# A three-part kernel in float32: table entries read earlier, the last expert's weights rounded in quarters, the last result in a bank of its own

## What is computed

```python
# experts: B=2, S=768, D=512, E=8, F=1024
for b in range(B):
    prev_e = -1
    for s in range(S):
        fresh_e = int(np.argmax(logits[b, s]))
        e = fresh_e if s == 0 or local_gate[b, s] < 0.5 else prev_e
        prev_e = e
        h = np.maximum(x[b, s] @ w1[e], 0.0)
        out[b, s] = p[e] * (h @ w2[e])
# mixing
theta = x @ w_theta
zr, zi = x * np.cos(theta), x * np.sin(theta)
y = einsum('ts,bsd->btd', w_tok_r, zr) + einsum('ts,bsd->btd', w_tok_i, zi)
u = x + y
out = u + np.maximum(u @ w_ch, 0.0)
```

## Time and profile before

| | us |
|---|---|
| median of 3 runs | 440.62 (440.28 to 440.92) |
| the profiled execution | 440.61 |
| its span, first to last instruction | 438.8 |
| TensorE busy (matmul) | 409.9 (93% of the span) |
| VectorE busy | 254.0 (58%) |
| ScalarE busy | 194.4 (44%) |
| GpSimd busy | 79.1 (18%) |
| mean granted TensorE clock | 0.977 of full speed |

### The profile page before, as it was taken

The page is one execution under the profiler, slowest core; times in us unless marked ns, Lnnn a source line. Parts: engine busy times, 40 slices in busy tenths (PEclk is TensorE's granted clock), DMA queues, the critical chain, the costliest instruction groups (busy, mean ns, idle before and its releaser), DMA issues.

```text
span 438.8 us, 8200 instructions
## 1 busy us (share of the span) xinstructions
PE 409.9 (93%) x2791; PEld 331.4 (76%) x2792; DVE 254.0 (58%) x403; ACT 194.4 (44%) x428; POOL 79.1 (18%) x128
## 2 busy tenths in 40 slices
PE   7779997299999999999999969999999999999997
PEld 3567786157888888888888758888888888888885
DVE  3898885786372624552215656566679465635252
ACT  1777994604264636473317564433333432123010
POOL 3776784121011111111030002500000000000000
PEclk9999999579999999999999989999999999999999
DMA  8999712927434521608140006400000000000012
GB/s 295 403 406 413 271 52 96 410 68 270 189 114 173 164 104 42 239 29 330 49 120 24 2 24 190 129 17 1 1 0 1 24 13 12 24 25 25 24 49 96
DMA packets 12541, 53.96 MB, mean 123 GB/s; under 512 B 1504, under 2 KB 1632, under 8 KB 10848
## 3 DMA queue, kind: packets, MB, share of 16 engines
q1 hardware_dynamic: 7680, 40.46, 23.9%
q0 software_dynamic: 2960, 9.70, 7.0%
q10 hardware_dynamic: 1872, 3.41, 2.0%
HBM read 40.46 MB, written 13.11 MB: 122 GB/s over the span
## 4 chain that ended last, share of the span: by engine, by line
PE 75%; DVE 4%; ACT 2%; issue 2%; ACTq 1%; POOL 1%; DVEq 0%; POOLq 0%
PE ps L1310 15%; PE ps L1312 14%; PE ps L1311 14%; PE ps L1457 7%; PE ps L1459 7%; PE ps L1458 7%; PE ps L1394 2%; PE ps L1358 2%; PE ps L1317 1%; PE ps L1305 1%; PE ps L1208 1%; ACT w_h L674 1%; DVE r_ol L952 1%; DVE w_l L985 1%; ACTq L664 1%
## 5 line engine op out<-in xcount | busy, mean ns | idle before, releaser
L1457 PE MATMUL ps<-z_h,mix_h 128*128 128x512 f32 x144 | 56.9, 395 | 0.0
L1459 PE MATMUL ps<-z_h,mix_l 128*128 128x512 f32 x144 | 56.1, 390 | 0.0
L1458 PE MATMUL ps<-z_l,mix_h 128*128 128x512 f32 x144 | 56.1, 390 | 0.0
L1310 PE MATMUL ps<-w_h,hT_h 128*128 128x512 f32 x104 | 42.6, 410 | 3.6 <-DVE hT_l L1004 3.3
L985 DVE TENSOR_TENSOR w_l<-w_raw,w_h (+1 forms) x32 | 37.2, 1221 | 11.9 <-ACT w_h L674 10.9
L618 ACT ACTIVATE p<-s,nmax 128x120 f32<-128x120 f32 x96 | 36.6, 387 | 12.2 <-DVE nmax L825 12.2
L1312 PE MATMUL ps<-w_l,hT_h 128*128 128x512 f32 x104 | 41.2, 396 | 0.0
L1311 PE MATMUL ps<-w_h,hT_l 128*128 128x512 f32 x104 | 41.1, 395 | 0.0
L1310 PE MATMUL ps<-w_h,xT_h 128*128 128x512 f32 x96 | 38.5, 401 | 0.6 <-DVE xT_l L998 0.6
L1312 PE MATMUL ps<-w_l,xT_h 128*128 128x512 f32 x96 | 37.5, 390 | 0.0
L1311 PE MATMUL ps<-w_h,xT_l 128*128 128x512 f32 x96 | 37.4, 390 | 0.0
(11 more groups left out here) (223 smaller groups left out, 850.1 us busy)
## 6 DMA issues: line engine op xcount, KB each, us to landing
w_raw<-w SPq DMA_DIRECT2D x8, 2048.0 KB, 9.0
mix_raw<-mix SPq DMA_DIRECT2D x1, 4608.0 KB, 14.0
ys<-zero SPq DMA_DIRECT2D x1, 3328.0 KB, 36.1
ys<-y_sb ACTq DMA_DIRECT2D x13, 256.0 KB
kfull<-k_full SPq DMA_DIRECT2D x8, 400.0 KB, 9.1
vpad<-v_pad SPq DMA_DIRECT2D x4, 768.0 KB, 12.2
xd<-x_sb POOLq DMA_DIRECT2D x12, 256.0 KB, 2.7
out<-o SPq DMA_DIRECT2D x12, 256.0 KB, 2.0
```

What stands on the lines that cost most here:

```text
L1310: pe.matmul(ps[:, bank, :], a_h[:, k, :], w_h[:, n, :], start=(k == 0), stop=False)
L1457: pe.matmul(ps[:, i, :], w_h, zh, start=(jb == 0 and m == 0), stop=False)
L1458: pe.matmul(ps[:, i, :], w_h, zl, start=False, stop=False)
L1459: mm = pe.matmul(ps[:, i, :], w_l, zh, start=False, stop=(jb == TPB - 1 and m == 1))
```

## The change

Three things are changed together, and a fourth goes with them.

1. ScalarE and VectorE read the four table entries of tiles 11 and 12 once, into registers, behind tile 0, and `split` takes them from there instead of reading the table each time.
2. Behind tile 11's last matmul ScalarE no longer copies and stores tile 11's result first; it waits for the matmul alone and rounds the first quarter of tile 12's second weights, then copies the transposed hidden rows, rounds the second quarter, makes the sines of the first mixing tile, and rounds the third and fourth quarter. VectorE follows in the same order: quarter, hidden rows, quarter, `z_product(0)`, two quarters.
3. Tile 12's second product goes to bank `B_YL` (bank 4, until then the bank of the transposed rows) instead of `B_Y` (bank 5), so that it needn't wait for the copy of tile 11's result. The two copies stand behind each other further down, the second into `h_sb`.
4. On VectorE the list of experts moves from ahead of the second tile's rows to behind tile 0's hidden rows (`list_experts`).

```diff
-            def split(t, raw, hi, arrived, done, a=0, b=STEPS):
-                place = place_of(t)
-                new = act.value_load(table[0:1, T_NEW, bass.ds(t, 1)], min_val=0, max_val=1)
+            def split(t, raw, hi, arrived, done, a=0, b=STEPS, known=None):
+                place, new = known or (place_of(t), is_new(t))
                 with act.If(new != 0):
...
             slot_tile(0, units=True, first=True)
+            known = [(place_of(n3 + i), is_new(n3 + i)) for i in (1, 2)]
+            w1_last = act.snap(known[1][0] * STEPS + 2 * STEPS)
...
-            split(t, w2_raw, w2_h, w2_in, w2_hi)
-            act.wait_ge(w1_split, place_of(t + 1) * STEPS + 2 * STEPS)
+            split(t, w2_raw, w2_h, w2_in, w2_hi, known=known[0])
+            act.wait_ge(w1_split, w1_last)
...
-            y_copy(t)
-            t = act.snap(n3 + 2)
-            split(t, w2_raw, w2_h, w2_in, w2_hi, 0, STEPS // 2)
-            hT_copy(t)
-            split(t, w2_raw, w2_h, w2_in, w2_hi, STEPS // 2, STEPS)
+            act.wait_ge(m2_done, t + 2)
+            act.sem_inc(passed_act, 1)
+            split(end, w2_raw, w2_h, w2_in, w2_hi, 0, 1, known[1])
+            hT_copy(end)
+            split(end, w2_raw, w2_h, w2_in, w2_hi, 1, 2, known[1])
             sines(0)
+            split(end, w2_raw, w2_h, w2_in, w2_hi, 2, STEPS, known[1])
             z_copy(0)
             turned(2)
             y_copy(t)
+            y_copy(end, bank=B_YL, y=y_last)
...
             def slot_tile(t, units=False, first=False):
                 hT_copy(t)
-                if not first:
+                if first:
+                    list_experts()
+                else:
                     split(t, w2_raw, w2_h, w2_l, w2_hi, w2_split)
                 xT_copy(t + 2)
...
-            split(t, w2_raw, w2_h, w2_l, w2_hi, w2_split, 0, STEPS // 2)
-            hT_copy(t)
-            split(t, w2_raw, w2_h, w2_l, w2_hi, w2_split, STEPS // 2, STEPS)
+            split(end, w2_raw, w2_h, w2_l, w2_hi, w2_split, 0, 1, known[1])
+            hT_copy(end)
+            split(end, w2_raw, w2_h, w2_l, w2_hi, w2_split, 1, 2, known[1])
             z_product(0)
+            split(end, w2_raw, w2_h, w2_l, w2_hi, w2_split, 2, STEPS, known[1])
             z_rest(0)
...
-            product2(t, place_of(t))
+            product2(t, place_of(t), bank=B_YL)
```

More of the change, by code:

```diff
@@ L689, in hT_copy, with y_copy @@
                        .then_inc(hT_hi, 1)
-            def y_copy(t, first=False):
+            def y_copy(t, first=False, bank=B_Y, y=y_sb[:, :]):
                 act.wait_ge(m2_done, t + 2)
-                if not first:
+                if not first and bank == B_Y:
                     act.wait_ge(y_stored, t * 16)
-                act.activation(y_sb[:, :], ps[:, B_Y, :], ACT.Copy).then_inc(y_taken, 1)
+                act.activation(y, ps[:, bank, :], ACT.Copy).then_inc(y_taken, 1)
                 act.wait_ge(y_taken, t + 1)
-                act.dma_start(ys_t[bass.ds(t, 1)], y_sb[:, :]).then_inc(y_stored, 16)
+                act.dma_start(ys_t[bass.ds(t, 1)], y).then_inc(y_stored, 16)
             act.wait_ge(table_ready, 1)
@@ L765, in _ @@
             turned(1)
-            relu(t + 1)
+            relu(end)
             x2_scale(2)
@@ L986, in split_step, with place_of, is_new, split @@
                                   hi[:, bass.ds(i * SW, SW), :].bitcast(f32), ALU.subtract).then_inc(done, 1)
-            def split(t, raw, hi, lo, hi_done, done, a=0, b=STEPS):
-                place = dve.value_load(table[0:1, T_PLACE, bass.ds(t, 1)], min_val=0, max_val=V - 1)
-                new = dve.value_load(table[0:1, T_NEW, bass.ds(t, 1)], min_val=0, max_val=1)
+            def place_of(t):
+                return dve.value_load(table[0:1, T_PLACE, bass.ds(t, 1)], min_val=0, max_val=V - 1)
+            def is_new(t):
+                return dve.value_load(table[0:1, T_NEW, bass.ds(t, 1)], min_val=0, max_val=1)
+            def split(t, raw, hi, lo, hi_done, done, a=0, b=STEPS, known=None):
+                place, new = known or (place_of(t), is_new(t))
                 with dve.If(new != 0):
@@ L1026, in _, with list_experts @@
             split(1, w1_raw, w1_h, w1_l, w1_hi, w1_split)
+            def list_experts():
+                link(dve.scalar_tensor_tensor(r_ord[:, E:V], r_used[:, E:V], r_last[:, 1:2], r_ord[:, E:V], ALU.add, ALU.subtract))
+                link(dve.tensor_tensor(r_te[:, 0:V, :], r_ord[:, :].unsqueeze(1).broadcast_to([1, V, V]),
+                                       const[0:1, C_TILE:C_TILE + V].unsqueeze(2).broadcast_to([1, V, V]), ALU.is_le))
+                link(dve.tensor_reduce(out=r_start[:, 0:V], in_=r_te[:, 0:V, :], op=ALU.add, axis=AX))
+                link(dve.tensor_scalar(r_tf[:, 0:V], r_start[:, 0:V], -1.0, V - 1.0, ALU.mult, ALU.add))
+                dve.tensor_tensor(table[0:1, X_EXPERT, 0:V], r_tf[:, 0:V], r_start[:, 0:V], ALU.min).then_inc(experts_ready, 1)
             def chosen():
@@ L1098, in _ @@
             t = dve.snap(n3 + 1)
+            end = dve.snap(n3 + 2)
             hT_copy(t)
-            split(t, w2_raw, w2_h, w2_l, w2_hi, w2_split)
+            split(t, w2_raw, w2_h, w2_l, w2_hi, w2_split, known=known[0])
             dve.wait_ge(wth_hi, 1)
@@ L1359, in transpose_h, with product2 @@
                 mm.then_inc(hT_ready, 1)
-            def product2(t, place, first=False, middle=None):
-                if not first:
+            def product2(t, place, first=False, middle=None, bank=B_Y):
+                if not first and bank == B_Y:
                     pe.wait_ge(y_taken, t)
@@ L1370, in product2 @@
                         pe.wait_ge(w2_split, place * STEPS + (STEPS + k // SW + 1))
-                    mm = product(B_Y, hT_h, hT_l, w2_h, w2_l, k, k, KF - 1)
+                    mm = product(bank, hT_h, hT_l, w2_h, w2_l, k, k, KF - 1)
                 mm.then_inc(m2_done, 1)
```

12 lines of the change are left out of this document (5 added, 7 removed).

## The result

The changed kernel takes 437.55 us in the median of 22 runs (435.00 to 441.42), the kernel before 440.94 (439.93 to 442.06). The ratio is 0.9926, with a 95% interval of 0.9908 to 0.9944. The direction is as predicted; a third of the gain is missing, and the runs spread over 6.4 us where the 22 of before, taken with them, spread over 2.1. (Runs of the kernel before that were taken later, 15 to 17 at a time, spread over 2.9 to 3.8.) The profiled execution took 438.15 with a span of 436.3, against 438.8 before.

A forecast was written before the change was run, and what follows sets the result against it. TensorE, with something in hand for 93% of the span, was taken as bound by where it waits. Seam 3.9 + start 0.6 + w_theta 0.6 = 5.1 us, so 440.6 - 5.1 = 435.5, range 434.4 to 437.6.

The forecast's parts named there:

- a lower clock: Rival at the seam: the clock falls in the new wait, costing 1.4 us, 436.9; shares chance 0.25 with two others.
- a late z: Rival at the seam: loop control delays the z operands, gain 3.7 in all, 436.9 to 437.5; within a shared 0.25.
- missing small gains: Rival: the two gains of 0.6, at the start and at w_theta, don't come, 436.7; within a shared 0.25.
- The seam: From tile 12's last four transposes to the first mixing matmul: mixing starts at 263.4 instead of 267.34, gaining 3.9 us.
- 0.6 for w_theta: In tile 11: table reads spared before ScalarE rounds w_theta let transposes and their rests come earlier, 0.6 us (bounds 0 and 1.0).
- The product's new wait: In tile 12's second product: TensorE waits about 1.0 us (0.7 to 1.3) for the third quarter of weights.
- z's rest: VectorE's last part of z before the first mixing matmul: ends at 263.0, just in time, with 0.4 us to spare.
- The start: Start of the expert stage: with the list moved, TensorE's wait for the second tile's rows goes, 0.6 us.
- Place 1's weights: Loads issued near 110.6, landing 119.8, no loss taken (bound 1.5); rival: late weights make it slower, chance 0.04.
- given back: Rival behind the seam: next mixing tiles' operands come late, up to 3 us return, 438.5; chance 0.08.
- the two places: TensorE's waits for VectorE's rests: 3.3 us for the hidden rows, 0.6 us for the second tile's rows.
- Nothing on the path: Behind tile 0: four table reads, 2.6 us on ScalarE, fall into its idle 3.73 in tile 1, costing nothing.

The follow-up runs named there:

- e7: e1 with the copy and store of tile 11's result back ahead of tile 12's first quarter; 436.61 us, 0.9898 of the kernel before.
- e8: e1 with the table entries read at each split again instead of held in registers; 437.43 us, 0.9928 of the kernel before.
- e11: The kernel before with ScalarE's four table entries held in registers and nothing else; 441.87 us, 1.0024 of the kernel before.
- e3: The kernel before with the move of the list of experts alone; 440.46 us, 0.9986 of the kernel before.
- e10: The changed kernel with the table entries read at each split again, row gathers as they were; 438.20 us, 0.9934 of the kernel before.
- e5: The kernel before with two unused table reads ahead of each row gather on GpSimd, making it later; 445.97 us, 1.0108 of the kernel before.
- e6: The kernel before with the slot entry copied ahead of GpSimd's wait, so gathers go out earlier; 440.77 us, 0.9993 of the kernel before.
- e9: e1 with the list of experts back at its old place; 436.34 us, 0.9907 of the kernel before.
- e1: The changed kernel with the slot entry copied ahead of GpSimd's wait for TensorE's transposes, so gathers go out earlier; 435.74 us, 0.9873 of the kernel before.
- e2: The changed kernel with the list of experts back at its old place; 437.36 us, 0.9919 of the kernel before.
- e4: The changed kernel with only a quarter of each later place's second weights loaded (512 KB instead of 2 MB); 435.94 us, 0.9883 of the kernel before.

## Why the prediction was half right

The time, 437.55, lies inside the stated range (434.4 to 437.6), 0.05 below its upper end, and that is luck. The part of the range above 436.2 was meant for a lower clock, a late z or missing small gains. In the traces none of these came; a loss that the sum doesn't have took their room.

**The seam** (3.9, with 0.6 for w_theta and the reads behind it): right in mechanism and size, 4.5 forecast and 4.7 measured. The end of tile 11's last matmul cuts it in two: 0.7 lies ahead of it (0.6 forecast), and from there to the mixing matmuls it took 10.4 instead of 14.5 us, 4.1 less (3.9 forecast). The product's new wait was put at 0.7 to 1.3, taken as 1.0, and is 0.68; the first quarter starts at 254.92, 0.43 behind the end of tile 11's last matmul (254.49), for the 0.5 forecast. z's rest, put 0.4 ahead of its need, is done at 264.21, 0.64 ahead of the first mixing matmul. By parts, the copy and store are worth 1.1 (e7) and the reads, with those at w_theta, 2.5 (e8; in e11 2.0 and 0.5 of clock). The remaining 1.1 of the 4.7 belongs to what was never taken out by itself: the new order of quarters, hidden rows and sines, the other bank, and the clock, whose share e3 puts at 0.5.

**The clock** stayed at 1.00 through the wait of 0.68 at the seam, and through the idle window 156 to 157. At the seam it stayed there in all traces with the first quarter moved forward, in e8 and e10 through a wait of 1.2, so the rival in which it drops there did not come true. The Trainium skill's page weighed there ("TensorE: Matmul & The Clock Gate", A second HAM failure mode) describes a swing that these stops at the seam don't show. But the length of a stop didn't settle it: behind 1.55 in e5 the clock fell, behind 3.3 in e3 it didn't, and behind the same 3.3 in before, e5 and e6 it did. So a late gather cost 1.6 us more in one execution than in another.

**The start**: 0.6 forecast, 0.8 in the stretches (137.6 to 136.8), 0.9 in e3 and e9. **Place 1's weights** went out at 109.97 for the 110.6 forecast, and cost nothing; that rival falls. The two loads landed one behind the other, not evenly shared: the last packet of the first ended at 118.5 (119.8 forecast), that of the second at 123.9, and ScalarE rounded from 121.02 without waiting for them. **The mixing stage** keeps its length, 171.5 and 171.4: what is gained in the seam reaches the end, and the rival "given back", as the prediction put it behind the seam, falls as well.

**The step that failed** is the sentence that closes the first part: away from the two places "what is gained there should reach the end, as long as nothing else arrives late". Its price of nothing for the held entries ("Nothing on the path", argued for the four reads behind tile 0) looked at where reads are added and at the seam, where they are spared. It didn't look at what ScalarE and VectorE do from tile to tile between the two once their turn is 0.2 shorter. What arrives late there is a gather that had 1.59 us of head start over 2 MB of weights and less than 1.1 to spare (e5). In the profiled execution this took back 3.4 us; by the medians of after and e1 it costs 1.8 (437.55 less 435.74). The smaller figure is what a toss-up at two places would give, and the runs' spread of 6.4 us fits it, the more so with a clock that falls behind some of the stops, but which copies were long in runs without a profile can't be seen.

The view that would have warned me is the timeline of GpSimd and SyncE in the kernel before, at 143 to 148: a gather and a large load 1.59 apart, with a copy of 0.29 that ends at a boundary of VectorE's. The growth of the copy could not be read there; that a small transfer with a deadline stood so close ahead of a large one could.

**Why 0.45 of head start is too little and 1.59 enough.** Over all traces the gather at 0.44 to 0.46 ahead of a full load was late in 6 of 6 places (two of after, one of e2, two of e5, one of e11), at 1.57 or more in none. The views of the transfer queues show a part of the reason. q1 carries the weights, q0 the gather; the rows have packets, MB and share of time. The changed kernel in 146 to 151 and in 151 to 157, then the kernel before in 148 to 151:

```profile
q1 hardware_dynamic: 74, 1.21, 67.4%
```

```profile
q1 hardware_dynamic: 70, 0.88, 42.0%
q0 software_dynamic: 80, 0.26, 14.6%
```

```profile
q1 hardware_dynamic: 34, 0.56, 59.2%
q0 software_dynamic: 80, 0.26, 38.8%
```

In the changed kernel 74 of the weights' packets go ahead of the gather's first one, though the gather was issued first; in the kernel before all 80 of the gather's go beside the first 34 of the weights. The records of the single packets give the times. The weights' first packet starts 0.95 to 1.34 us behind their instruction. The gather's starts 1.7 to 2.4 behind its own at head starts of 1.57 and more, and 4.9 to 5.1 in the six late places; from its first to its last packet it takes 1.2 to 2.2 us in the one case and 4.4 to 5.6 in the other. So with 0.45 of head start the weights are on the transfer engines first, with 1.57 the gather is. An estimate from these figures: the order turns at a head start of 0.5 to 0.9; no run has one between 0.46 and 1.57.

The Trainium skill ("DMA: Bandwidth & Descriptors", Queues, rings and completion order) states that each transfer engine takes turns between its queues, a packet at a time. The two queues in the changed kernel's window 145 to 160 are

```profile
q1 hardware_dynamic: 144, 2.10, 39.3%
q0 software_dynamic: 80, 0.26, 5.9%
```

An estimate from these rows: five packets of the gather on each of 16 engines, each behind one of the weights' packets of 14.6 KB, wait for 1.17 MB, 3.3 us at the 350 GB/s that the rows come to (2.36 MB in 45.2% of 15 us). From its first to its last packet the gather took 5.6 us instead of 2.0 in the first place and 4.5 instead of 1.4 in the second, 3.6 and 3.1 more: the rule has the right size for this part.

**What stays open** is the other part, 3.1 us in each place: why the gather's first packet starts 5.0 behind its instruction instead of 1.9 once the weights are ahead of it. No run here separates that.

## What to carry to other kernels

An edit to one engine's stream can shift it against every other engine, even in a loop that the edit doesn't touch (here by 0.2 us); before pricing it at nothing, look for transfers that arrive just in time, and above all for a small one that is issued shortly ahead of a large one. Whatever prepares such a transfer (here the copy of a slot entry) belongs ahead of the wait that releases it: three lines that were worth nothing in the kernel before (e6) are worth 1.8 us behind the change (e1, 0.9873 of before, the best version here). And when a changed kernel's runs spread much wider than before (here 6.4 us against 2.1 to 3.8), some race between engines may be decided differently from run to run: look for a wait in the profile that isn't in all executions.

## What the runs showed of the hardware

- A GpSimd copy of 128x1 numbers behind the transposes took 0.18 to 0.29 us, or 1.28 to 1.29 in 5 of the 8 cases in which it came 0.05 to 0.07 ahead of the end of a VectorE rounding of 1.16 us with another rounding behind it (after, e2, e4, e11). The instruction of the gather takes 0.97 alone and 1.14 to 1.70 beside such roundings.
- A gather of 256 KB had landed within 3.9 to 5.1 us with a head start of 2.0 to 2.1 over a load of 2 MB (e1, e6, e7, e8, e9), and landed in 9.7 to 11.0 with one of 0.45 (after, e2, e5, e11). Its first packet then started 4.9 to 5.1 us behind its instruction, against 1.7 to 2.4 at head starts of 1.57 and more. With a load of 0.5 MB behind it, at the same 0.45, no one waited for it (e4, one case).
- A TensorE stop of 1.48 for rows costs 2.2, since the next weight loads and matmuls start up 0.57 late behind it. The granted clock stayed at 1.00 behind that one and fell to 0.50 behind one of 1.55 (e5), which cost 1.6 more; behind a stop of 3.3 it fell in before, e5 and e6 and not in e3.
